# Causal window attention and two expert layers on one core: the first batch with unpadded keys, a second set of input buffers, and its normalization and most of its bias on GpSimd

## The reference

```python
def _attn_ref(q, k, v):                       # (4, 8, 576, 64) each
    scores = scale * np.matmul(q, k.transpose(0, 1, 3, 2))
    rel = pos[:, None] - pos[None, :]
    bias = slopes[:, None, None] * (-np.abs(rel))[None, :, :]
    mask = (rel >= 0) & (rel < 128)
    scores = np.where(mask, scores + bias[None], -1000000000.0)
    scores = scores - np.max(scores, axis=-1, keepdims=True)
    attn = np.exp(scores)
    attn = attn / (np.sum(attn, axis=-1, keepdims=True) + 1e-09)
    return np.matmul(attn, v)
def _moe_ref(x, w_in, w_out):                 # x is (2304, 512), hidden 2048
    r = np.maximum(x @ w_in, 0.0)
    return (r * r) @ w_out
def _moe2_ref(x, w_gate, w1, w2):             # 8 experts, hidden 1024
    ...                                       # gate: softmax numerator, 8 row and column scalings
    for e in range(E):
        out += P[:, e:e + 1] * (np.maximum(x @ w1[e], 0.0) @ w2[e])
```

## Time and profile before

| | us |
|---|---|
| median of three executions | 2125.3 |
| lowest, highest | 2122.79, 2128.08 |
| the profiled execution, its own time | 2127.54 |
| span of the profiled execution, first to last instruction | 2125.8 |
| PE busy, share of the span | 98% |
| DVE, ACT, POOL busy | 62%, 39%, 58% |
| TensorE clock granted, mean over the span | 0.995 |

### The profile page before, as it was taken

One profiled execution on the slowest core, in us unless ns is written; L12 is line 12 of the kernel. 1 busy time (PEld: TensorE's weight loads), 2 busy tenths in 40 slices (PEclk: granted clock), 3 DMA queues, 4 the chain that ended last, 5 costly groups with the idle time before them and its releaser, 6 DMA issues.

```text
span 2125.8 us, 37567 instructions
## 1 busy us (share of the span) xinstructions
PE 2085.9 (98%) x11906; PEld 1881.9 (89%) x11906; DVE 1310.8 (62%) x2729; ACT 821.1 (39%) x1643; POOL 1227.6 (58%) x1604
## 2 busy tenths in 40 slices
PE   7899999999999999999999999999999999999999
PEld 3799898899998998999988999899998999989898
DVE  7566665676657655565665655556566565655655
ACT  5565565564532332333332323333333333323332
POOL 3122322224457666666776666666676766676663
PEclk9999999999999999999999999999999999999999
DMA  5232332322222122222222222222222222222221
GB/s 125 67 83 61 99 85 78 88 78 60 85 65 60 61 69 69 69 69 69 67 63 98 65 64 69 69 69 69 68 66 94 70 69 66 64 67 69 69 69 60
DMA packets 208145, 154.55 MB, mean 73 GB/s; under 512 B 66464, under 2 KB 164768, under 8 KB 208032
## 3 DMA queue, kind: packets, MB, share of 16 engines
q1 hardware_dynamic: 208032, 153.15, 24.7%
HBM read 148.39 MB, written 4.72 MB: 72 GB/s over the span
## 4 chain that ended last, share of the span: by engine, by line
PE 92%; DVE 3%; issue 2%; ACT 1%; POOL 1%; DMA 0%; SPq 0%; DVEq 0%; ACTq 0%; POOLq 0%
PE bank L788 36%; PE bank L749 32%; PE bank L688 10%; PE bank L681 9%; PE bank L646 2%; PE bank L672 1%; PE bank L657 1%; DVE relu L1156 1%; ACT prob L884 1%; DVE prob L1089 0%; PE bank L617 0%; DVE prob L1119 0%; POOL el L564 0%; DVE g1l L1131 0%; DVE gl L1232 0%
## 5 line engine op out<-in xcount | busy, mean ns | idle before, releaser
L564 POOL TENSOR_TENSOR el<-ew,eh 128x256 fp32r<-128x256 f32 x672 | 471.8, 738 | 293.5 <-ACT eh L852 293.5
L1275 DVE SCALAR_TENSOR_TENSOR z_sb<-bank,gate,z_sb 128x512 f32<-128x512 f32 x540 | 403.7, 749 | 248.1 <-PE bank L788 248.1
L749 PE MATMUL bank<-xh,eh 128*128 128x384 f32 x1344 | 451.0, 336 | 3.5 <-DVE gl L1232 3.5
L749 PE MATMUL bank<-xh,el 128*128 128x384 f32 x1344 | 450.8, 335 | 0.0
L788 PE MATMUL bank<-fh,gh 128*128 128x512 f32 x1152 | 450.4, 391 | 0.4 <-DVE z_sb L1275 0.4
L788 PE MATMUL bank<-fh,gl 128*128 128x512 f32 x1152 | 450.7, 391 | 0.0
L788 PE MATMUL bank<-fl,gh 128*128 128x512 f32 x1152 | 450.5, 391 | 0.0
L749 PE MATMUL bank<-xl,eh 128*128 128x384 f32 x1344 | 450.3, 335 | 0.0
L502 POOL TENSOR_TENSOR wl<-stage,wh 128x512 fp32r<-128x512 f32 x120 | 159.8, 1332 | 372.8 <-ACT wh L852 372.8
L574 POOL TENSOR_TENSOR fl<-fw,fh 128x256 fp32r<-128x256 f32 x384 | 274.4, 746 | 133.6 <-ACT fh L852 133.3
L852 ACT ACTIVATE p<-bank 128x384 f32<-128x384 f32 x96 | 47.2, 492 | 654.0 <-PE bank L749 654.0
(11 more groups left out here) (130 smaller groups left out, 2985.4 us busy)
## 6 DMA issues: line engine op xcount, KB each, us to landing
fw<-in_moe_w_dram SPq DMA_DIRECT2D x96, 512.0 KB, 3.6
ew<-in_moe_w_dram SPq DMA_DIRECT2D x96, 256.0 KB, 2.8
stage<-in_moe_w_in_dram SPq DMA_DIRECT2D x64, 256.0 KB, 3.0
stage<-in_moe_w_out_dram SPq DMA_DIRECT2D x64, 256.0 KB, 2.8
a<-in_moe_w_dram SPq DMA_DIRECT2D x96, 128.0 KB, 2.7
ew<-in_moe_w_dram SPq DMA_DIRECT2D x96, 128.0 KB, 2.9
k_raw<-in_k_dram SPq DMA_DIRECT2D x32, 128.0 KB, 2.7
q_raw<-in_q_dram SPq DMA_DIRECT2D x32, 128.0 KB, 2.5
```

The lines of the kernel that those rows point to most:

```text
L564: last = pool.tensor_tensor(el[r][:, a, :, :], ew[r][:, a, :, :], f(eh[r][:, a, :, :]), ALU.subtract)
L749: done = pe.matmul(ps, w[r][:, a, kc, :], x[:, b, kc, :], start=(first and kc == 0 and w is eh and x is xh), stop=(kc == 1 and w is el), s ...
L1275: dve.scalar_tensor_tensor(out=z, in0=ps, scalar=weight, in1=z, op0=ALU.mult, op1=ALU.add).then_inc(z_free, 1)
```

## The change

In the first stage only:

- The keys are not padded. `kT0` replaces `kz0` (one copy instead of one for each head), and the scores come from two matmuls of 64 rows and 256 columns, head 0 from partitions 0 to 63 into `s_ps`, head 1 from partitions 64 to 127 into `s_odd`, which are two more PSUM banks.
- ACT copies all 128 rows of k; DVE has no part in round 0. Each transpose round now waits for `t_lo` and `t_hi`.
- Odd pairs have input buffers of their own, `k_odd` and `q_odd`. SP issues the loads of pair 1 right behind those of pair 0, ahead of the first weights, and that of pair c+2 after the last transposes of pair c.
- POOL makes six of the eight bias tiles, after DVE's two, from a `dist` buffer of its own, and multiplies the probabilities by their reciprocals (`normalize`), in slot j for step j-1, ahead of the weight piece of that slot.
- DVE makes both parts of the output (`o_lo`); ACT no longer makes the rounded copy (`o_hi`) in this stage.

```diff
@@ -108,7 +108,11 @@
-        kz0 = sb("kz0", [P, 2, 2, QT * P], fp32, placed["qT0"])
+        kT0 = sb("kT0", [P, 2, QT * P], fp32, placed["qT0"])
+        q_odd = sb("q_odd", [P, QT, 2, D], fp32, placed["kT0"])
+        k_odd = sb("k_odd", [P, QT, 2, D], fp32, placed["q_odd"])
+        dist = sb("dist", [P, 2 * P], fp32, placed["k_odd"])
+        assert placed["dist"] <= W0 + 4 * WS
@@ -381,7 +387,10 @@
             def stretch(events, b, n0, u0, last):
...
-                    if what == "round" and a[1] == ROUNDS - 1 and a[0] + 1 < KC:
+                    if what == "round" and a[1] == ROUNDS - 1 and plain(b) and a[0] + 2 < KC:
+                        sp.wait_ge(t_done, (a[0] + 1) * ROUNDS)
+                        load_alone(a[0] + 2)
+                    if what == "round" and a[1] == ROUNDS - 1 and not plain(b) and a[0] + 1 < KC:
@@ -399,8 +408,13 @@
-            load(0, k_raw, kf, k_in)
-            load(0, q_raw, qf, q_in)
+            def load_alone(c):
...
+                load(c, (k_raw, k_odd)[c % 2], kf, (k_in, k_odd_in)[c % 2])
+                load(c, (q_raw, q_odd)[c % 2], qf, (q_in, q_odd_in)[c % 2])
...
+            load_alone(0)
+            load_alone(1)
@@ -484,17 +498,30 @@
-            dist = prob[:, 0, 0, :]
...
-            link(pool.iota(dist, pattern=[[1, 2 * P]], base=-P, channel_multiplier=-1,
+            link(pool.iota(dist[:, :], pattern=[[1, 2 * P]], base=-P, channel_multiplier=-1,
...
-            link(pool.affine_select(out=dist, in_=dist, compare_op=ALU.is_ge, fill=deep,
+            link(pool.affine_select(out=dist[:, :], in_=dist[:, :], compare_op=ALU.is_ge, fill=deep,
...
-            pool.affine_select(out=dist, in_=dist, compare_op=ALU.is_ge, fill=deep, base=WINDOW - 1 - P,
+            pool.affine_select(out=dist[:, :], in_=dist[:, :], compare_op=ALU.is_ge, fill=deep, base=WINDOW - 1 - P,
...
+            pool.wait_ge(dist_ready, 1)
+            pool.wait_ge(bias_ready, 2)
+            for h in range(2, H):
+                pool.tensor_scalar(bias[:, h, :], dist[:, :], float(2.0 ** (-8.0 * (h + 1) / H)), MASKED,
+                                   ALU.mult, ALU.max).then_inc(bias_ready, 1)
...
+            def normalize(j):
...
+                nq, k0 = span(j % QT)
+                pool.wait_ge(dve_chain, 2 * j + 2)
+                for h in range(2):
+                    p = prob[0:nq, j % 2, h, k0:]
+                    last = pool.tensor_scalar(p, p, rinv[0:nq, j % 2, h:h + 1], None, ALU.mult)
+                last.then_inc(norm_done, 1)
@@ -527,6 +554,8 @@
             def stretch(events, n0, u0):
...
+                    if what == "slot" and u0 == 0 and 0 <= a[0] - 1 < STEPS:
+                        normalize(a[0] - 1)
@@ -603,21 +632,26 @@
         def _(pe):
...
-            pe.wait_ge(zeros_ready, 3)
+            pe.wait_ge(zeros_ready, 2)
...
             def transpose_round(b, c, r):
+                k_now, q_now = (k_odd, q_odd) if plain(b) and c % 2 else (k_raw, q_raw)
+                if r < 2 and plain(b):
+                    pe.wait_ge(((k_in, q_in), (k_odd_in, q_odd_in))[c % 2][r], 3 * 16 * (c // 2 + 1))
+                elif r < 2:
+                    pe.wait_ge((k_in, q_in)[r], b * (3 * 16 * KC) + 3 * 16 * (c + 1 - KC // 2))
+                if not isinstance(b, int) or c or r:
...
+                    wait_alone(pe, t_lo, b * (ROUNDS * KC) + (ROUNDS * c + r))
+                    if plain(b):
+                        pe.wait_ge(t_hi, ROUNDS * c + r)
...
-                    pe.wait_ge((k_in, q_in)[r], b * (3 * 16 * KC) + 3 * 16 * (c + 1))
-                if not isinstance(b, int) or c or r:
...
-                    wait_alone(pe, t_lo, b * (ROUNDS * KC) + (ROUNDS * c + r))
-                if r < 2:
-                    raw = (k_raw, q_raw)[r]
+                    raw = (k_now, q_now)[r]
...
-                    for i, raw in enumerate((q_raw, k_raw)):
+                    for i, raw in enumerate((q_now, k_now)):
@@ -635,13 +669,19 @@
+                if plain(b) and t in (0, FULL):
+                    pe.wait_ge(t_hi, ROUNDS * c + (2 if t == 0 else 3))
...
+                if plain(b):
+                    for h in range(2):
+                        d = slice(h * D, (h + 1) * D)
+                        last = pe.matmul((s_ps, s_odd)[h][j % n][:, k0:2 * P], qT0[d, s, t * P:(t + 1) * P],
+                                         kT0[d, s, (t - 1) * P + k0:(t + 1) * P], start=True, stop=True)
+                    last.then_inc(s_done, 1)
+                    return
...
-                if plain(b):
-                    products = ((qT0[:, s, :], kz0[:, s, :, :]),)
-                else:
-                    products = ((qTh, kzh), (qTh, kzl), (qTl, kzh))
+                products = ((qTh, kzh), (qTh, kzl), (qTl, kzh))
@@ -858,12 +898,10 @@
-                        return
-                    o, i = (slice(0, FULL * P), slice(0, FULL * P)) if r == 0 else (slice(FULL * P, S), slice(TAIL, 2 * TAIL))
-                    for h in range(2 if r else 1):
-                        d = slice(h * D, (h + 1) * D)
-                        last = copy(kz0[d, s, h, o], t_ps[d, i])
-                    last.then_inc(t_hi, 1)
+                    elif r == 0:
+                        copy(kT0[:, s, 0:FULL * P], t_ps[:, :]).then_inc(t_hi, 1)
+                    else:
+                        copy(kT0[:, s, FULL * P:S], t_ps[:, TAIL:2 * TAIL]).then_inc(t_hi, 1)
@@ -941,7 +979,7 @@
-                        if 0 <= j - OUT_LAG < STEPS:
+                        if 0 <= j - OUT_LAG < STEPS and not plain(b):
@@ -1041,13 +1079,11 @@
         def _(dve):
...
-            for r in range(2):
-                dve.memset(kz0[:, r, :, :], 0.0).then_inc(zeros_ready, 1)
+            dve.memset(kT0[:, :, FULL * P:], 0.0).then_inc(zeros_ready, 1)
...
-            for h in range(H):
-                dve.tensor_scalar(bias[:, h, :], prob[:, 0, 0, :], float(2.0 ** (-8.0 * (h + 1) / H)), MASKED,
+            for h in range(2):
+                dve.tensor_scalar(bias[:, h, :], dist[:, :], float(2.0 ** (-8.0 * (h + 1) / H)), MASKED,
...
-            dve.wait_ge(bias_ready, H)
@@ -1058,14 +1094,13 @@
-                    dve.wait_ge(t_done if r == 1 else t_hi, b * (ROUNDS * KC) + (ROUNDS * c + r + 1))
...
-                        last = dve.tensor_copy(kz0[D:2 * D, s, 1, 0:FULL * P], t_ps[D:2 * D, :])
-                    else:
-                        at = slice(0, FULL * P) if r == 1 else slice(FULL * P, S)
-                        last = dve.tensor_scalar(qT0[:, s, at], t_ps[:, 0:FULL * P if r == 1 else TAIL],
-                                                 SCALE, None, ALU.mult)
-                    last.then_inc(t_lo, 1)
+                        dve.sem_inc(t_lo, 1)
+                        return
+                    dve.wait_ge(t_done if r == 1 else t_hi, ROUNDS * c + r + 1)
+                    at = slice(0, FULL * P) if r == 1 else slice(FULL * P, S)
+                    dve.tensor_scalar(qT0[:, s, at], t_ps[:, 0:FULL * P if r == 1 else TAIL],
+                                      SCALE, None, ALU.mult).then_inc(t_lo, 1)
@@ -1122,6 +1163,9 @@
             def o_lo(b, j):
...
+                if plain(b):
+                    dve.wait_ge(pv_done, j + 1)
+                    dve.tensor_copy(x_part(b, 0, c, t, nq), o_ps[:, 0:nq]).then_inc(x_hi, 1)
```

More of the change, by code:

```diff
@@ L174, in attention_moe_moe_kernel @@
         bank = [ctx.enter_context(nc.psum_tensor(f"bank{i}", [P, 512], fp32)) for i in range(8)]
-        s_ps, pT_ps = [bank[0], bank[4]], [bank[1], bank[5]]
+        s_ps, s_odd, pT_ps = [bank[0], bank[4]], [bank[6], bank[7]], [bank[1], bank[5]]
         o_ps, t_ps = bank[2], bank[3]
@@ L196, in attention_moe_moe_kernel @@
         k_in = sem("k_in")
+        q_odd_in = sem("q_odd_in")
+        k_odd_in = sem("k_odd_in")
         v_in = [sem(f"v_in{r}") for r in range(2)]
@@ L1088, in biased @@
                     wait_alone(dve, s_done, b * STEPS + (j + 1))
+                if plain(b) and h == 0 and j % QT == 0:
+                    dve.wait_ge(bias_ready, 2 * (j // QT) + 2)
+                scored = (s_ps, s_odd)[h][j % n][0:nq, k0:2 * P] if plain(b) else \
+                    s_ps[j % n][0:nq, h * 2 * P + k0:(h + 1) * 2 * P]
                 last = dve.tensor_tensor_reduce(
-                    out=prob[0:nq, j % 2, h, k0:], in0=s_ps[j % n][0:nq, h * 2 * P + k0:(h + 1) * 2 * P],
+                    out=prob[0:nq, j % 2, h, k0:], in0=scored,
                     in1=bias[0:nq, 2 * (j // QT) + h, k0:], scale=-1.0, scalar=3.0e38,
```

## The result

| | before | after |
|---|---|---|
| median, us | 2125.9 (6 runs) | 2144.9 (6 runs) |
| ratio after to before | | 1.0089, 95% interval 1.0076 to 1.0102 |
| span of the profiled execution | 2125.8 | 2142.8 |
| first matmul of the second stage starts at | 69.57 | 87.84 |
| from there to the end | 2056.2 | 2055.0 |

What follows compares the result with a forecast made beforehand. The first stage was taken as bound by a chain from engine to engine, the rest by PE. Start 2.2, second pair's inputs 0.8, steps 0.0 and last normalization -0.1 gave 2.9 us gained: median 2122.4, range 2115.5 to 2129.5.

Steps and rivals of the forecast that it cites:

- The price of POOL's multiplication: First-stage normalization on POOL: 0.40 us for each head's multiplication, 0.80 for both, with bounds of 0.36 and 0.74.
- The ring: Dependency round of one first-stage step, reciprocals through normalization, transposes and next bias addition: 2.45 us, before 2.36.
- Rival (2): POOL's multiplication costs 0.74 us, like a subtraction of tensors; steps 10.4 us longer, time 2132.8; chance 12%.
- the turning point: Price of one POOL multiplication, about 0.50 us, at which 3.4 us more on the steps uses up the gain.
- The clock: Rival: PE idler in the first stage, three half-clock falls of three steps, 3.6 us, 2126.0; 13% shared with rival (3).
- The drain: End of the first stage: the last normalization costs 0.1 us more on POOL than on DVE.
- The start: Before step 0: q's transposes begin 2.0 us earlier, tails' copy saves 0.2; first bias addition near 10.0, not 12.17.
- the six bias tiles: Start of the first stage: made on POOL, first needed by step 5, over 10 us later, so no cost.
- The second pair's inputs: Early loads of pair 1 end PE's wait for its keys between steps 1 and 2: 0.8 us gained.
- The weight pieces: POOL's pieces in every second slot delay steps 2 to 19: seven at 0.6 us each, 4.2 us.
- rival (3): DVE's sums meet every weight piece: 4.2 us worse than the forecast, 2126.6; 13% shared with the clock rival.
- DVE's output copy: In each first-stage step DVE copies the output, 0.28 us; its wait for PE's product is met by 0.4 us.

Runs made afterwards that it cites:

- run 4: The changed kernel with one two-tensor multiplication on POOL for both heads in place of two by a value for each row: 2129.6 us, ratio 1.0021.
- run 3: The kernel before with nothing changed but the normalization, moved from DVE to POOL: 2142.3 us, ratio 1.0087.
- run 5: The changed kernel with each pair of score matmuls issued twice, same result: 2150.6 us, ratio 1.0114.
- run 9: The changed kernel with normalization back on DVE, plus 160 PE instructions that do no work in the first stage: 2133.8 us, ratio 1.0045.
- run 6: The changed kernel with all eight bias tiles on DVE and none on POOL: 2142.5 us (median of three), ratio 1.0078.
- run 10: The changed kernel with normalization and all eight bias tiles back on DVE: 2127.8 us, ratio 1.0007.
- run 11: The changed kernel with normalization back on DVE and pair c+1 loaded only after pair c's transposes: 2127.2 us, ratio 1.0007.
- run 1: The changed kernel with the normalization back on DVE, all else kept: 2123.6 us, ratio to before 0.9997.
- run 2: The changed kernel with normalization back on DVE and the output's rounded copy back on ACT: 2128.4 us, ratio 1.0014.

## Why the prediction was wrong

**The price of POOL's multiplication: the step that failed.** It was taken as 0.40 us, "the nearest row", the selection of the same shape, with bounds of 0.36 and 0.74. It measured 0.92, outside them. The upper bound rested on the thought that an instruction with one tensor can't be dearer than one with two. On this engine it is: 0.92 for 256 columns against 0.61 for 256 and 1.04 for 512 in the two-tensor form (run 4).

**The ring itself held.** With N for the two multiplications the prediction had 1.65 + N. At 1.82 that is 3.47; 3.43 was measured, and 3.42 in run 3. At 1.04 it is 2.69; 2.62 was measured. Rival (2), "the multiplication costs on POOL what a subtraction of tensors does", had the mechanism, the place and the turning point of 0.50, at 12%, but its end, 2132.8, was too low because its price was a bound that did not bound. With the measured 1.82 the prediction's own sum is 17 x 3.47 - 0.75 = 58.2 us for the steps; run 5, with no long transposes, measured 58.5.

**The clock** was a rival's term, "three falls of three steps". It was larger: granted at half from about 42 to 52 and 59 to 93 us, no faster than that up to 38 us by the durations of the transposes, and 14 of 17 groups of transposes long (the rival had nine, 3.6 us), 3.2 us on the steps by run 3 and 4.1 by run 5, and part of the 2.2 in the drain. Given the longer ring, PE did less per microsecond. That the idleness is the cause was only argued; run 9 speaks against a simple form of it.

**The drain** was a term of 0.1 us, "the last normalization". It lengthened by 2.2 (run 3: by 2.0). The last four multiplications stand behind each other on POOL for 3.65 us, and the clock was at half:

```profile
78.92 3.65 POOL L523 TENSOR_SCALAR prob<-prob,rinv 128x256 f32<-128x256 f32 x4 [2.05 <-DVE rinv L1151]
```

**The start:** 2.2 us forecast, 2.6 measured. The first addition was put at about 10.0 and came at 9.56. But that the six bias tiles "are first needed by step 5 and cost nothing" was wrong: I asked who needs the tiles, and not what is queued behind them. They took 6.8 us, the first normalization waited for POOL, and 1.7 us were lost at step 2 (run 6).

**The second pair's inputs:** 0.8 us forecast. In the changed kernel nothing of it showed (4.56 us from step 1 to step 2); with the bias alone back on DVE it was 2.82 (run 6). With normalization and bias on DVE (run 10) the interval is 2.30 for 3.20, 0.9 us. Over the whole stage the early loads are worth 1.1 us by one trace of each kernel (run 11).

**The weight pieces:** 0.6 us each, 4.2 in all. In the changed kernel they ran while PE transposed and cost little; with the short ring of run 4 an interval with a piece is mostly 2.79 to 2.90 and once 3.05 for 2.62, so 0.2 to 0.4. The collision of rival (3) is real where DVE does the multiplications: 2.11 for 0.61 (run 1). The rule weighed in the prediction, from the Trainium skill (SBUF — State Buffer, "Who interferes with whom"), is that the loser stands for the whole of the other's instruction. The trace agrees as far as it goes: the pair needs 0.61 us and ended 0.16 after the last POOL instruction, so it stood for 1.5 of the 1.9 us of the two.

**DVE's output copy** was costed at nothing, and no run shows a cost (run 2).

## What to carry to other kernels

When an operation moves to an engine on which no row shows it, a row of another operation there is no bound, not even a seemingly harder one; the range has to be wider, or the turning point (here 0.50 us) has to carry the chances. Ask for each moved instruction what stands behind it in its new queue, not only who needs its result. And where a change adds or removes instructions ahead of a loop, compare the stretches behind the edit before reading the total. Read PE's pace from the duration of one kind of instruction, not from the granted clock alone.

## What the hardware showed that I had not expected

- On POOL a tensor-scalar instruction of 256 columns takes 0.85 us (one operation, a constant), 0.92 (a value for each row) and 1.07 (two operations, constants). A selection of the same shape takes 0.40 and a cast of 512 columns 0.61. The two-tensor multiplication with the value broadcast takes 0.61 for 256 and 1.04 for 512.
- 64 rows cost as much as 128 there (0.916 and 0.922 us).
- A granted clock of 1.00 is no measurement ahead of the first level that the trace has on record. In the changed kernel that is at 38.5 us; up to 38 us four transposes took 1.08 to 1.09 us, as they did later at a granted 0.50. In run 5, with the scores doubled, they took 0.63 from 18.6 us on.
- The place of PE's loop in its instruction stream is worth about 10 us: 2052.2 us behind the first stage in run 1, 2064.0 with 160 more instructions ahead of it, 2055.9 with 256. A page of the Trainium skill has a mechanism that would do this (Runtime: NRT & Kernel Launch, "Instruction fetch mechanics"): instructions come in blocks of 256, and a taken branch to a place outside the blocks that are held has to wait for their fetch. The trace agrees with the 256, as far as these shifts go, and shows the idle time near the turns of the loop; no run here shows the fetch itself.
